# Convolution and two MLPs on one core: x moved by DMAs in other slots, the rest of the result summed by GpSimd, four tiles ahead of the loop

## The reference

```
w = softmax(weight, axis=-1)                    # 8 heads, 7 taps
x1[t] = sum_k w[head, k] * x[t - 6 + k]         # causal, per head of 24 channels
h = x1 @ w_in                                   # 192 x 2048
g = where(h >= 1, h, where(h <= -1, 0, (h + 1)**2 / 4))
x2 = g @ w_out                                  # 2048 x 192
h = x2 @ w_in2
out = (h / (1 + exp(-1.702 * h))) @ w_out2      # 8192 x 192
```

## Time and profile before

| what | value |
|---|---|
| median of 3 runs | 1173.59 us (1173.38 to 1175.2) |
| the profiled execution, its own time | 1176.4 us |
| its span, first to last instruction | 1174.6 us |
| mean granted TensorE clock | 0.999 |
| busy PE, PEld, DVE, ACT, POOL | 1146.1, 1011.3, 844.6, 799.3, 432.3 us |
| instructions PE, PEld, DVE, ACT, POOL | 9382, 9382, 1206, 1510, 425 |
| DMA packets, bytes | 63857, 31.27 MB, 9.6% of 16 engines' span |

### The profile page before, as it was taken

How to read it: one execution, slowest core, us unless ns; L and a number is a source line. 1 busy time by engine, 2 the same in 40 slices (tenths; PEclk the granted TensorE clock), 3 DMA queues, 4 the chain that set the end, 5 groups by cost and what they waited for, 6 DMA issues and landing times.

```text
span 1174.6 us, 25920 instructions
## 1 busy us (share of the span) xinstructions
PE 1146.1 (98%) x9382; PEld 1011.3 (86%) x9382; DVE 844.6 (72%) x1206; ACT 799.3 (68%) x1510; POOL 432.3 (37%) x425
## 2 busy tenths in 40 slices
PE   7999999999999999999999999999999999999998
PEld 4767898998988889888888889889898888999987
DVE  6877768686776868768686786867768686676633
ACT  4866676767758677686766767677686766855554
POOL 5897626080440805327071350905317071000000
PEclk9999999999999999999999999999999999999999
DMA  6312101001010000101001010010101000000001
GB/s 193 97 37 75 35 1 48 1 10 40 1 48 1 15 35 2 47 1 48 2 8 41 1 49 1 12 37 1 49 1 48 1 7 9 2 15 2 14 2 28
DMA packets 63857, 31.27 MB, mean 27 GB/s; under 512 B 56084, under 2 KB 60562, under 8 KB 63760
## 3 DMA queue, kind: packets, MB, share of 16 engines
q1 hardware_dynamic: 63760, 29.80, 9.6%
HBM read 23.09 MB, written 6.29 MB: 25 GB/s over the span
## 4 chain that ended last, share of the span: by engine, by line
PE 73%; DVE 8%; ACT 8%; issue 5%; POOL 4%; SPq 1%; DMA 0%; DVEq 0%; ACTq 0%; POOLq 0%
PE acc_all L764 3%; PE acc_all L756 2%; PE acc_all L742 2%; PE acc_all L761 2%; PE acc_all L759 2%; PE acc_all L767 2%; DVE g_lo L1115 2%; PE h_all L697 2%; PE h_all L699 2%; PE h_all L694 2%; ACT clip L938 2%; PE h_all L701 2%; PE h_all L703 2%; PE acc_all L738 2%; PE acc_all L740 2%
## 5 line engine op out<-in xcount | busy, mean ns | idle before, releaser
L1115 DVE TENSOR_TENSOR g_lo<-gate,g_hi 128x512 fp32r<-128x512 f32 x232 | 205.1, 884 | 92.2 <-ACT g_hi L944 87.3
L1121 DVE TENSOR_TENSOR g_lo<-h_all,g_hi 128x512 fp32r<-128x512 f32 x256 | 175.7, 686 | 124.8 <-ACT h_all L955 122.5
L944 ACT ACTIVATE g_hi<-gate 128x512 fp32r<-128x512 f32 x232 | 146.5, 632 | 166.2 <-DVE gate L1109 131.4
L938 ACT ACTIVATE clip<-clip,half 128x512 f32<-128x512 f32 x256 | 184.9, 722 | 60.5 <-DVE clip L1100 58.0
L952 ACT ACTIVATE g_hi<-h_all 128x512 fp32r<-128x512 f32 x256 | 152.9, 597 | 94.6 <-PE h_all L705 66.7
L510 POOL TENSOR_TENSOR x_conv<-x_in,tap_w 128x384 f32<-128x384 f32 (+1 forms) x29 | 24.7, 872 | 515.9 <-ACT raw L990 513.4
L1100 DVE TENSOR_SCALAR clip<-h_all 128x512 f32<-128x512 f32 x256 | 174.9, 683 | 20.8 <-PE h_all L703 17.3
L517 POOL TENSOR_TENSOR x_conv<-x_conv,prod 128x384 f32<-128x384 f32 (+1 forms) x174 | 187.5, 1098 | 1.6
L1109 DVE TENSOR_TENSOR gate<-h_all,clip 128x512 f32<-128x512 f32 x232 | 160.5, 692 | 35.7 <-ACT clip L938 24.1
L510 POOL TENSOR_TENSOR prod<-x_in,tap_w 128x384 f32<-128x384 f32 (+1 forms) x174 | 176.4, 1038 | 4.2
L955 ACT ACTIVATE h_all<-h_all 128x512 f32<-128x512 f32 x256 | 151.6, 592 | 0.0
(11 more groups left out here) (281 smaller groups left out, 4763.2 us busy)
## 6 DMA issues: line engine op xcount, KB each, us to landing
x_in<-in_x SPq DMA_DIRECT2D x14, 960.0 KB, 4.7
out_y<-raw SPq DMA_DIRECT2D x360, 16.0 KB, 1.4
raw<-in_moe_w_out SPq DMA_DIRECT2D x6, 384.0 KB, 3.5
raw<-in_moe_w_in SPq DMA_DIRECT2D x4, 512.0 KB, 4.5
raw<-in_moe_w_in SPq DMA_DIRECT2D x8, 256.0 KB, 4.8
stage<-in_moe_w_out SPq DMA_DIRECT2D x2, 384.0 KB, 7.4
x_in<-in_x SPq DMA_DIRECT2D x1, 768.0 KB, 8.7
x_in<-in_x SPq DMA_DIRECT2D x2, 283.5 KB
```

The lines of the kernel that those rows point to most:

```text
L938: nc.scalar.activation(c, c, ACT.Square, bias=half[:, :], scale=0.5).then_inc(square_ready, 1)
L944: nc.scalar.activation(g1_hi[step.s % G_RING][:, :], gate1_of(step)[:, :], ACT.Copy).then_inc(g1_hi_ready, 1)
L1115: nc.vector.tensor_tensor(g1_lo[k][:, :], gate1_of(step)[:, :], g1_hi[k][:, :].bitcast(FP32), ALU.subtract).then_inc(g1_lo_ready, 1)
L1121: nc.vector.tensor_tensor(g2_lo[k][:, :], bank2(step)[:, :], g2_hi[k][:, :].bitcast(FP32), ALU.subtract).then_inc(g2_lo_ready, 1)
```

## The change

- ACT's move_x is gone. SP issues 24 DMAs per tile instead, in the order load(tile + 2), move(tile + 1), store(tile - 2). A move waits for the convolution of its tile and for the turns of the tile before.
- The tables of slots: EARLY (tiles of the loop, and tile 3) turns x in 4 and 5, rounds in 5 and 6, splits in 7 and 8. MIDDLE (tile 2): turns 8 and 10, rounds 9 and 10, splits 13 and 14. LATE (tile 1): both turns and both roundings in 13, both splits in 14, and in DVE's slot these come behind L1100 instead of ahead of L1115.
- GpSimd's convolution starts when the moves have landed, x_in is loaded and, from tile 3 on, the split of the next tile's x is done.
- ACT copies the whole rest accumulator in slot 8 and in slot 9 its upper half again, from SBUF to partitions 0 to 63 (out_shift, in y_part). GpSimd adds the two (sum_out) after the third multiply of its convolution; PE waits for ACT's copies (out_copied) and not for the sum.
- The turns of the result stand in slots 11 and 12. take_y part 2 of DVE is in slot 3.
- HEAD_TILES is 4: tiles 2 and 3 are straight code, the loop has five passes (tiles 4 to 13). Waits of PE for the last weight chunks, written for the loop (LAST_CHUNKS), fall away, since the straight code has its own.

```diff
-        out_rest, rest_turned = raw[3][0:DR, 0:TT], raw[3][0:DR, TT:2 * TT]
+        out_both, out_rest, rest_turned = raw[3][:, 0:TT], raw[3][0:DR, 0:TT], raw[3][0:DR, TT:2 * TT]
+        out_shift = y_part[0:DR, :]
...
-        HEAD_TILES = 2
-        LOOP_PAIRS = PAIRS - 2
+        HEAD_TILES = 4
+        LOOP_PAIRS = PAIRS - 1 - HEAD_TILES // 2
...
-        EARLY = dict(move={3: [0], 4: [1], 5: [2], 6: [3], 7: [4], 9: [5]}, turn={8: [0], 11: [1]},
-                     hi={10: [0], 11: [1]}, lo={12: [0], 13: [1]})
-        LATE = dict(move={}, turn={13: [0], 14: [1]}, hi={13: [0], 14: [1]}, lo={14: [0], 15: [1]})
+        EARLY = dict(turn={4: [0], 5: [1]}, hi={5: [0], 6: [1]}, lo={7: [0], 8: [1]})
+        MIDDLE = dict(turn={8: [0], 10: [1]}, hi={9: [0], 10: [1]}, lo={13: [0], 14: [1]})
+        LATE = dict(turn={13: [0, 1]}, hi={13: [0, 1]}, lo={14: [0, 1]})
...
+            def move(tile):
+                sp.wait_ge(conv_step, tile * CONV_STEPS)
+
+                sp.wait_ge(x_turn_done, (tile - 2) * 2)
+                move_x(range(MOVES))
+
+            for tile in range(2, HEAD_TILES):
+                load(tile + 2)
+                move(tile + 1)
+                store(tile - 2)
             with nc.Fori(0, LOOP_PAIRS, engines=(sp.engine,), hint_back_edge=True) as i:
                 for tile, side in loop_tiles(i):
                     load(tile + 2)
+                    move(tile + 1)
                     store(tile - 2)
+            move(TILES - 1)
...
+            def sum_out(tile):
+                pool.wait_ge(out_shifted, tile + 1)
+                nc.gpsimd.tensor_tensor(out_rest, out_rest, out_shift, ALU.add).then_inc(out_summed, 1)
...
+                    if result is not None and k == 2:
+                        sum_out(result)
...
+            def prepare(tile):
+                pool.wait_ge(main_x_moved, tile * moves_landed(0))
+                pool.wait_ge(rest_x_moved, tile * moves_landed(1))
+                pool.wait_ge(x_loaded, (tile + 3) * 16)
+                if not isinstance(tile, int) or tile > 2:
+                    pool.wait_ge(x_from_dve, (tile + 2) * 2)
+                convolve(tile + 2, slabs=2, result=tile - 2)
...
-                    pe.wait_ge(out_summed, two.tile)
+                    pe.wait_ge(out_copied, two.tile * 2)
...
-                else:
-                    nc.scalar.activation(out_rest, rest[DR:P, :], ACT.Copy).then_inc(out_copied, 1)
+                elif part == 1:
+                    nc.scalar.activation(out_both, rest[:, :], ACT.Copy).then_inc(out_copied, 1)
+                else:
+                    act.wait_ge(out_copied, (tile + 1) * 2)
+                    nc.scalar.activation(out_shift, out_both[DR:P, :], ACT.Copy).then_inc(out_shifted, 1)
...
+                if takes_out(tile) and s == OUT_SLOT + 1:
+                    take_out(tile - 2, 2)
                 if prepares(tile):
                     at = prep(tile)
-                    for group in at["move"].get(s, ()):
-                        move_x(tile + 1, group)
...
-            def sum_out(tile):
-                dve.wait_ge(out_copied, tile * 2 + 2)
-                nc.vector.tensor_tensor(out_rest, acc2[1][0:DR, :], out_rest, ALU.add).then_inc(out_summed, 1)
...
-                if takes_y(tile) and not solo and at_y == 2:
+                if takes_y(tile) and not solo and at_y == 3:
                     take_y(tile - 1, 1 - side, 2)
-                if takes_out(tile) and s == OUT_SLOT + 6:
+                if takes_out(tile) and s == OUT_SLOT + 3:
                     turn_main(tile - 2)
-                if takes_out(tile) and s == OUT_SLOT + 7:
+                if takes_out(tile) and s == OUT_SLOT + 4:
                     turn_rest(tile - 2)
...
+                if is_late(tile):
+                    prepare_x(tile, side, s)
                 if two is not None:
                     residue2(two)
```

More of the change, by code:

```diff
@@ L286, in conv_mlp_mlp, with is_late @@
         OUT_SLOT = (BEHIND + 1 - 1) % F_TILES
-        EARLY = dict(move={3: [0], 4: [1], 5: [2], 6: [3], 7: [4], 9: [5]}, turn={8: [0], 11: [1]},
-                     hi={10: [0], 11: [1]}, lo={12: [0], 13: [1]})
-        LATE = dict(move={}, turn={13: [0], 14: [1]}, hi={13: [0], 14: [1]}, lo={14: [0], 15: [1]})
+        EARLY = dict(turn={4: [0], 5: [1]}, hi={5: [0], 6: [1]}, lo={7: [0], 8: [1]})
+        MIDDLE = dict(turn={8: [0], 10: [1]}, hi={9: [0], 10: [1]}, lo={13: [0], 14: [1]})
+        LATE = dict(turn={13: [0, 1]}, hi={13: [0, 1]}, lo={14: [0, 1]})
+        def is_late(tile):
+            return isinstance(tile, int) and tile == 1
         def prep(tile):
-            return LATE if isinstance(tile, int) and tile == 1 else EARLY
+            if is_late(tile):
+                return LATE
+            return MIDDLE if isinstance(tile, int) and tile == 2 else EARLY
         CHUNKS = [("main", 0), ("rest", 0), ("out", 0), ("out", 1),
@@ L520, in conv_ops, with convolve @@
                 return multiply, add
-            def convolve(tile, slabs, between=None):
+            def sum_out(tile):
+                pool.wait_ge(out_shifted, tile + 1)
+                nc.gpsimd.tensor_tensor(out_rest, out_rest, out_shift, ALU.add).then_inc(out_summed, 1)
+            def convolve(tile, slabs, between=None, result=None):
                 multiply, add = conv_ops(tile, slabs=slabs)
@@ L593, in _ @@
             convolve(3, slabs=2)
+            def prepare(tile):
[5 more added lines that the diff above has]
+                convolve(tile + 2, slabs=2, result=tile - 2)
+            for tile in range(2, HEAD_TILES):
+                prepare(tile)
             with nc.Fori(0, LOOP_PAIRS, engines=(pool.engine,), hint_back_edge=True) as i:
                 for tile, side in loop_tiles(i):
-                    pool.wait_ge(x_moved, (tile - 1) * MOVES)
-                    pool.wait_ge(x_loaded, (tile + 3) * 16)
-                    convolve(tile + 2, slabs=2)
+                    prepare(tile)
+            for tile in range(TILES - 4, TILES - 1):
+                sum_out(tile)
         @block.tensor
@@ L803, in down2 @@
                 if first:
-                    pe.wait_ge(out_summed, step.tile)
+                    pe.wait_ge(out_copied, step.tile * 2)
                 nc.tensor.matmul(rest[:, :], w_rest, hi[:, :], start=first, stop=False)
@@ L981, in take_x @@
                 nc.scalar.activation(rest[DR:P, :], banks[1][DR:P, :], ACT.Copy).then_inc(x_from_act, 1)
[L983 to L993, removed]
             def round_x(tile, side, part):
@@ L1158, in turn_x @@
                 rows = slice(0, P) if part == 0 else slice(DR, P)
-                moved = DM // BLOCK if part == 0 else MOVES
+                dve.wait_ge(main_x_moved if part == 0 else rest_x_moved, (tile - 1) * moves_landed(part))
                 if isinstance(tile, int) and tile == 2:
-                    dve.wait_ge(main_x_moved if part == 0 else rest_x_moved, moves_landed(part))
                     dve.wait_ge(wp_ready, RAW_ORDER[1][-1] + 1 - DVE_CHUNKS)
-                else:
-                    dve.wait_ge(x_moved, (tile - 3) * MOVES + moved)
                 nc.vector.transpose(x_turned[part][rows, :], x_blocks[part][rows, :]).then_inc(x_turn_done, 1)
@@ L1191, in split_weights, with prepare_x @@
                 nc.vector.tensor_tensor(lo, raw_view(n)[:, cols], hi.bitcast(FP32), ALU.subtract).then_inc(w_ready, 1)
+            def prepare_x(tile, side, s):
+                at = prep(tile)
+                for part in at["turn"].get(s, ()):
+                    turn_x(tile + 1, part)
+                for part in at["lo"].get(s, ()):
+                    split_x(tile + 1, 1 - side, part)
             def slot(tile, side, s):
@@ L1197, in slot @@
                 at_y = s - shift_y(tile)
-                if takes_y(tile) and not solo and at_y == 2:
+                if takes_y(tile) and not solo and at_y == 3:
                     take_y(tile - 1, 1 - side, 2)
-                if takes_out(tile) and s == OUT_SLOT + 6:
+                if takes_out(tile) and s == OUT_SLOT + 3:
                     turn_main(tile - 2)
-                if takes_out(tile) and s == OUT_SLOT + 7:
+                if takes_out(tile) and s == OUT_SLOT + 4:
                     turn_rest(tile - 2)
[L1205 to L1210, removed]
+                if prepares(tile) and not is_late(tile):
+                    prepare_x(tile, side, s)
                 if takes_y(tile) and not solo and s == 1:
```

7 lines of the change are left out of this document (1 added, 6 removed).

## The result

The changed kernel takes 1157.36 us, median of 4 runs (1156.24 to 1158.17); the kernel before, run with it, 1174.2. The ratio is 0.9861, 95% interval 0.9849 to 0.9874: 16.8 us faster, with 1157.7 forecast. The profiled execution took 1157.41 us, with a span of 1155.7.

A forecast was written before the change was run, and what follows sets the result against it. PE, busy 98%, was taken as the bound, losing time to DVE's residue. Savings of 13.7 (tiles 3 to 14), 0.7 (tile 15) and 1.5 (tile 2) made 15.9: 1160.5 profiled, 1157.7 against the median; range 1154.5 to 1167.5.

The forecast's parts named there:

- take_y part 2: DVE's part 2 of y, moved from slot 2 to 3, stops waiting for y_rest: 9.1 us in tiles 3 to 15, 1.5 in tile 2.
- Where the loss was: Tiles 3 to 14: excess of 17.5 us over 4.333 us slots, mostly PE waiting for DVE's gate 1 residue; 13.7 saved.
- the exit's 0.8 us stays: At the loop's exit: PE's 0.8 us idle was expected to remain with tiles 2 and 3 outside the loop.
- it was x that was awaited there: Start of tile 2: PE's 1.4 us idle was put down to x, so moving the loop's entry was taken as 0.
- By themselves they are worth nothing: ACT's moves in slots 3 to 9: removing 7.4 us per tile gains nothing there; their cost is missing lead in slot 11.
- ACT's load was not the cause: Rival: slot 12 keeps its 0.7 in four odd tiles, 2.8 us back, 1160.5; inside the forecast, no separate chance.
- The quiet slots: Turns and splits of x go to slots 4 to 8, ahead of the convolution, where residues take 0.69 us.
- The rule against it: VectorE instructions with two SBUF inputs contend with GpSimd reading SBUF; moving the sum to GpSimd would lengthen the blocking.
- the first rival: Block meets the result's turns: slot 11 or 12 loses 0.7 in each of twelve tiles, 8.4 back, 1166.1; chance 0.12.
- Not late: GpSimd's convolution waits for ACT's shift of slot 9 some 8 us after its start in slot 8: no delay.
- The late-moves rival: SP's moves land late, blocking turns of x in slots 4 and 5 past 8.7 us to spare: 1197.7; chance 0.05.
- Entry 0: Loop's entry, now at tile 4: cost between 0 and 1.4 us, taken as 0.

The follow-up runs named there:

- ACT's load kept: The changed kernel with four idle ACT copies of 32x128 put back in each of slots 3, 4, 5, 6, 7 and 9: 1170.39 us, ratio 0.9961.

## Why the prediction was right, step by step

**Where the loss was.** Right. Tiles 3 to 14 gave back 849.5 - 833.6 = 15.9 us of the 17.5, for 13.7 forecast. Two terms were too cautious. The 3.0 left for y_part and small ones came to 833.6 - 832.0 = 1.6: a weight load's wait of 0.26 lengthens its slot by less, as the prediction said of the others and did not apply here. And "the exit's 0.8 us stays" was wrong: no idle time at the exit, nor in the run that moved take_y's slot alone. What makes it come and go is open. The 6.1 us that remain beside take_y's slot in these tiles were forecast as 13.7 less twelve times 0.70, 5.3.

**take_y part 2.** Right in mechanism and size: the 9.1 + 1.5 us forecast for it lie between the 9.9 of doing it alone and the 11.2 of undoing it.

**Tile 2** gave 2.2, from 72.3 to 70.1 us, for 1.5: a slot of 6.13 in the run with take_y back in slot 2 is 4.33 in the change and so gave 1.8 alone: the upper bound of 1.9 was the better value. Tile 15 gave its 0.7, tile 1 and the tail nothing together. The idle time at the start of tile 2, which "it was x that was awaited there" explained, went from 1.4 to 1.1 us only, although the last split of x ends at 115.8 and the matmul starts at 117.2 in the changed kernel; PE's own record names DVE's L1132 as the releaser there. So x was not all that was awaited; the 0 taken for tile 1 came out right, but not by the account given for it.

**The sum against the two times.** 15.9 was forecast from the profiled execution and its span fell by 1174.6 - 1155.7 = 18.9. The forecast of the profile, 1160.5, was 3.1 too high. The predicted median, 1157.7 for 1157.36, is nearer than that because the profiled execution of before lay 2.8 us above its median and the one of after lies on its own. That two such differences of 3 us cancel is luck; the terms themselves were 3 us too cautious.

**"By themselves they are worth nothing" (ACT's moves).** PE did keep its 4.33 us beside them, and load on ACT does cost where turns and roundings come on top: six loaded slots cost 9.7 us in the twelve tiles. The prediction tied the cost to slot 11, behind slot 9's moves. Whether that place was right is open: four copies in slot 10 alone cost nothing, and with six loaded slots 0.4 us are lost before slot 9's copies run, but the roundings of x stand in two of those slots. The rival "ACT's load was not the cause" wanted slot 12 to keep its 0.7 us in four odd tiles; it takes 4.33 us in all twelve. But the turn of x has left slot 11 too, so that alone doesn't name ACT. The old slots without ACT's moves, which would have settled it, were not run.

**The quiet slots.** With ACT relieved, x turned and split beside the convolution costs at most 1 us in the twelve tiles (834.6 for 833.6), so the alignment with GpSimd is the small part of the 6.1 there. What remains for the rest is ACT's relief and the order of DVE's work in slots 11 to 14; no run shows how they share it.

**The rule against it.** The residue behind each turn of the result, with GpSimd at work, takes 1.25 and 1.20 us instead of 0.69. The Trainium skill (SBUF — State Buffer, Who interferes with whom) says that a VectorE instruction with two SBUF inputs contends with a GpSimd instruction that reads SBUF; the rows agree. So the first rival's collision does happen in tile 6, and costs nothing: PE's slots are 4.33 us. The prediction's reason was that no waiting ACT stands ahead of it. That fits the run with ACT's load kept, where the same slots of tile 6 show waits again (slot 12 takes 4.69 us), but it was not tested by itself.

**"Not late" (GpSimd waits for the shift).** Wrong, harmlessly: GpSimd waits 1.82 us (at the sum's row), so the convolution with its sum takes 463.8 - 434.2 = 29.6 us, for 28.4 reckoned. That and little else brings the margin of the moves from 8.7 to 8.1. The late-moves rival had its place, and its point of decision at 8.7 us, right; its price of one for one was measured as 8.6 for 8.6.

**The loop.** "Entry 0" holds in the changed kernel; alone, the same edit cost 2.4 us, which the prediction had no term for.

## What to carry to other kernels

Look for an instruction that waits on another engine while standing in front of the one that feeds the busiest engine: moving it one slot was one number and gave more than half of the gain. Judge a helper engine's load by whether it still waits for the bound engine in each slot, not by its busy share: four copies in slot 10 were made up by the next slot; 24 copies over six slots, with two roundings among them, were not. Before work goes on a queue, work out when it is wanted in every stage, the first tiles too: 8 us of margin hid 8 more DMAs (about 5 us) in the twelve tiles, and of the 16.7 us of 24 more it hid 8 and let the rest through to PE.

## What the runs showed of the hardware

**Long blocking.** A DVE instruction with two SBUF inputs was twice seen to last over several GpSimd instructions in a row. DVE in tile 2 of the run with 8 more moves:

```profile
169.16 3.58 DVE L1140 TENSOR_TENSOR g_lo<-gate,g_hi 128x512 fp32r<-128x512 f32 x1
```

GpSimd in the same microseconds:

```profile
168.31 1.28 POOL L545 TENSOR_TENSOR raw<-raw,y_part 64x512 f32<-64x512 f32 x1
169.57 1.68 POOL L531 TENSOR_TENSOR prod<-x_in,tap_w 128x384 f32<-128x384 f32 x2
171.21 2.40 POOL L538 TENSOR_TENSOR x_conv<-x_conv,prod 128x384 f32<-128x384 f32 x2
```

It takes 3.58 us instead of 0.69, from 169.16 to 172.74: the end of L545, both L531 and most of the pair of L538, and PE's slot 12 there lasts 6.39 us. The 8 more DMAs of the tile make its convolution start at 160.51 instead of 155.38 us, so that the sum (L545) now runs beside the turn of the result and the residue behind it; that is a path by which more DMAs reach PE without a late move. In the profiled execution with ACT's load kept an instruction took 7.57 us in the head, where GpSimd worked without a break until 77.70:

```profile
70.68 7.57 DVE L1167 TENSOR_TENSOR y_rest_a<-y_part,y_rest_a 64x512 fp32r<-64x512 f32 x1
```

That execution took 1174.9, against its median of 1170.39. What decides when DVE gets its turn was not tried.

**Gaps without a releaser.** DVE's 2.72 us marked issue (the run with four tiles outside the loop) has its like in other variants, 2.0 us on DVE at the residue of gate 1 in both runs with the sum on DVE, and neither of the two kernels compared has one there. They come and go with edits elsewhere, so differences of about 1 us above are read from the twelve tiles and not from the median. In the run with load in slot 10, one of 1.3 us stands on ACT. What causes them is open.

**The clock after a stall.** While PE waited for the late move of tile 2, the granted clock fell from 1.00 (135 to 139 us) to 0.82 in the window of the wait, in which PE was busy for 3.03 of 10 us, and was 0.50 (1.2 of 2.4 GHz) in the 4 us after it. PE's weight load waited 8.9 us, but the slot was 15.48 - 4.33 = 11.15 us longer; PE shows no other wait in it.
